# Layer one's first unit in another order on three engines, and a later wait for the low parts of the weight sums

## The chip, the cores and the metric

The kernel runs on one core of one Trainium2 chip. The metric is the device time of one execution in microseconds. Engines are named as in the profile: PE is TensorE (PEld its weight loads), DVE is VectorE, ACT is ScalarE, POOL is GpSimd, SP issues the DMAs.

## The reference

A hash-bucketed attention (2 batches, 8 heads, 768 tokens, head size 64), then two gated MLPs.

```python
def _attn_ref(q, k, v, proj):
    ...
    mask = q_bucket[:, :, :, None] == k_bucket[:, :, None, :]
    scores = np.where(mask, scale * q @ k.T, -1e9)
    attn = exp(scores - max); attn = attn / (sum(attn) + 1e-09)
    return attn @ v
def _moe_ref(x, w1, w2, w3, w_out):        # 1536 x 512, width 1024
    return ((x @ w1) * (x @ w2) @ w3) @ w_out
def _moe2_ref(x, w_gate, w_val, w_out):    # 1536 x 512, width 1536
    return (sigmoid(x @ w_gate) * (x @ w_val)) @ w_out
```

All is float32. The kernel splits each float32 operand into a high part (rounded to the matmul's format, fp32r) and a low part (the rest), and makes each product from three matmuls: high by high, low by high, high by low.

## The kernel before, in words

The work has four stages: attention over eight pairs of heads (0 to about 281 us), layer one (`x @ w1` and `x @ w2`, gated, to about 404 us), layer two (w3 times w_out), and layer three with the last product (to 746.9 us).

Layers one and three use a Strassen-like scheme with seven products for each 2 x 2 block of blocks. A unit is one block column of one weight matrix: `unit(pair, j)` with j = 0 for the first matrix and j = 1 for the second. Seven products follow each other, each for two sides (halves of the tokens): B11, T3, T2, T1, B22, B21, T4, named after the operand from x. B names are blocks of x, T names are sums of blocks. The product of one side is six matmuls of 128x384. Each product needs the operand's high and low part and the weight's high and low part. The weights A11, A12, A22 are raw blocks; S1 to S4 are sums of blocks. B11, B21 and T4 use raw blocks, T3, T2, T1 and B22 use sums.

Around the first unit the order is written out by hand, with counting semaphores:

- GpSimd, for each unit, runs `pair_sums` (four sums, L549 to L557), `pair_raw_low` (L562, signals `g_raw_split`) and `pair_sums_low` (L567, signals `g_ready`). For unit 1 this follows its last work for attention, the low parts of B22 (L634). `pair_sums(1, 1)` waits for the weights' load and for the last attention-side product of weights (`wp_done`).
- ScalarE runs `pair_raw_high` and `pair_sums_high` for the weights' high parts, `x_operand_high` for the operands' high parts, and `kept1`, `kept2`, `kept4`, which copy a bank of partial results to memory after the products B11, T2 and T1. TensorE waits for the copy of one side before it goes on in the same bank (T2, T1 and B22 wait for `u1_kept`, `u2_kept`, `u4_kept`). Its order for the first unit stands from L868 to L887.
- VectorE makes the operands' low parts (`x_operand_low`, L1070, two inputs in SBUF, signals `x_ready`), the last attention results (`attention_out`, L1054), the sums for T4 (`x_sum4_begin`, `x_sum4`) and, within `unit`, adds a bank to a kept part (L1184). The T3 low parts stand at the end of the last pair (L1128, L1129), ahead of the last `transposed_lo` (L1048), which makes `pt_lo`. The order behind stands from L1164 to L1178. The T4 low parts follow the first two adds of unit 0 (L1232).
- TensorE ends attention with the last value products, whose last twelve matmuls (`values`, L1351) stand between B11 and T3 of the first unit; they need all `pt_lo`. At its start a unit waits for `g_ready`, that is for all low parts of its weights.
- SP loads the next weights (`load_pair`, L424) when GpSimd has finished the raw low parts of the unit before.

Of the kernel before, what the change touches and what calls it, by code (L numbers as in the profile page):

```python
# [65 lines left out]
B11, T3, T2, T1, B22, B21, T4 = range(7)  # L66
# [4 lines left out]
X_LOW_ORDER = ((T3, 0), (T3, 1), (T2, 0), (T2, 1), (T1, 0), (T1, 1), (B21, 0), (B21, 1), (T4, 0), (T4, 1))  # L71
# [9 lines left out]
def build(nc, qk_d, v_d, proj_d, shift_d, w1_d, w2_d, w3_d, wo1_d, wg_d, wv_d, wo2_d, out_d):  # L81
    ctx = ExitStack()
    with ctx:
# [117 lines left out]
        u_x, u_y = kept_parts(1, (86, 89, 92)), kept_parts(3, (134, 137, 161))  # L201
# [57 lines left out]
        x_hi_done, x_ready = sem("x_hi_done"), sem("x_ready")  # L259
# [218 lines left out]
        def _(pool):  # L478
# [63 lines left out]
            def pair_sums(unit, j):  # L542

                sums = g_sum[j]
                pool.wait_ge(g_loaded, 48 * (unit + 1))
                at_least(pool, w2_mm, 2 * (unit - 1))
                if isinstance(unit, int) and unit == 1:
                    pool.wait_ge(wp_done, PAIRS)
                pool.tensor_tensor(sums[:, S1 - S1, :], g_raw21[:, 0, :], g_raw[:, A22, :],  # L549
                                   ALU.add).then_inc(g_sums_done, 1)  # L550
                pool.tensor_tensor(sums[:, S3 - S1, :], g_raw[:, A11, :], g_raw21[:, 0, :],
                                   ALU.subtract).then_inc(g_sums_done, 1)
                pool.wait_ge(g_sums_done, 4 * unit + 1)
                pool.tensor_tensor(sums[:, S2 - S1, :], sums[:, S1 - S1, :], g_raw[:, A11, :],
                                   ALU.subtract).then_inc(g_sums_done, 1)
                pool.wait_ge(g_sums_done, 4 * unit + 3)
                pool.tensor_tensor(sums[:, S4 - S1, :], g_raw[:, A12, :], sums[:, S2 - S1, :],  # L557
                                   ALU.subtract).then_inc(g_sums_done, 1)
# [126 lines left out]
        def _(act):  # L685
# [3 lines left out]
            def pair_raw_high(unit, j):  # L689

                act.wait_ge(g_loaded, 48 * (unit + 1))
                at_least(act, w2_mm, 2 * (unit - 1))
                if isinstance(unit, int) and unit == 1:
                    act.wait_ge(wp_done, PAIRS)
                copy(g_hi[j][:, A11:S1, :], g_raw[:, :, :]).then_inc(g_raw_hi_done, 1)
# [5 lines left out]
            def x_operand_high(q, side):  # L701

                if q == T1:
                    act.wait_ge(s_done, STEPS * PAIRS)
                if q in (T2, T1):
                    act.wait_ge(x_sums_done, {T2: 3, T1: 5}[q] + side)
                    act.wait_ge(s_done, STEPS * (PAIRS - 1) + QT)
                if q == B21:
                    act.wait_ge(wp_done, PAIRS)
                    act.wait_ge(x_done, 2 * PAIRS - 1 + 2 * side)  # L710
                if q == T4:
                    act.wait_ge(x_sum4_begun, 1)
                    act.wait_ge(x_sum4_done, side + 1)
                copy(x_high(q, side), x_raw(q, side)).then_inc(x_hi_done, 1)
# [114 lines left out]
            def kept2(pair, j, side, u):  # L829
                kept(pair, j, side, y2_mm, u2_kept, u[1], g21_done, v21_done)  # L830

            def kept4(pair, j, side, u):
                kept(pair, j, side, y3_mm, u4_kept, u[2], g22_done, v22_done)
# [33 lines left out]

            x_take_t2()  # L868
            kept1(0, 0, 0, u_x)
            pair_raw_high(1, 1)  # L870
            kept1(0, 0, 1, u_x)
            x_operand_high(T1, 1)
            attention_halves(3, PAIRS - 1, keep=False)
            kept2(0, 0, 0, u_x)
            x_operand_high(B21, 0)
            kept2(0, 0, 1, u_x)
            x_operand_high(B21, 1)
            kept4(0, 0, 0, u_x)
            kept4(0, 0, 1, u_x)
            x_operand_high(T4, 0)  # L880
            x_operand_high(T4, 1)
            for side in range(2):
# [113 lines left out]
        def _(dve):  # L996
# [103 lines left out]
            def pair(p, first=False, last=False):  # L1100
                for k in range(STEPS):
                    nxt = None if last and k == STEPS - 1 else (p, k + 1) if k + 1 < STEPS else (p + 1, 0)
                    if nxt:
                        row_max(*nxt)
                    if last:
                        sum_eps(p, k)
                    if nxt:
                        exp_scale(*nxt)
                    if last:
                        inverse(p, k)  # L1110
                    if nxt:
                        exp_bias(*nxt)
                    if last and k not in NORM_ON_ACT:
                        normalise(p, k)
                    if k == 0 and not first:
                        sums_eps_of(p - 1, 1)
                    if k > 0:
                        transposed_lo(p, k - 1)
                    elif not first:
                        inverse_of(p - 1)  # L1120
                        transposed_lo(p - 1, STEPS - 1)
                        turn(p - 1)
                    if k == QT and not last:
                        sums_eps_of(p, 0)
                    if k == (4 if first else 2) and not last:
                        code(p + 1)
                    if last and k == STEPS - 1:
                        x_operand_low(T3, 0)  # L1128
                        x_operand_low(T3, 1)  # L1129

            dve.memset(inverses[:, :], 0.0).then_inc(pad_set, 1)
            dve.wait_ge(pad_set, 1)
# [29 lines left out]
                pair(p)  # L1162
            pair(PAIRS - 1, last=True)
            transposed_lo(PAIRS - 1, STEPS - 1)  # L1164
            x_sum4_begin()
            x_operand_low(T2, 0)
            x_operand_low(T2, 1)
            dve.wait_ge(x_kept, 4 * PAIRS - 1)
            attention_out(slice(0, 2 * D), 0, x_f[:, PAIRS - 1, 0:HALF])
            x_sum4(0)  # L1170
            x_operand_low(T1, 0)
            x_operand_low(T1, 1)
            attention_out(slice(0, D), 1, x_f[0:D, PAIRS - 1, HALF:SEQ])
            dve.wait_ge(x_tmp_done, 4 * PAIRS)
            attention_out(slice(D, 2 * D), 1, pv_bank[D:2 * D, 0:HALF])
# [130 lines left out]
        def _(pe):  # L1306
# [129 lines left out]
            def unit(pair, j, high, low, operand=None, behind_first=()):  # L1436


                n = 4 * pair + 2 * j
                pe.wait_ge(g_ready, 2 * pair + j + 1)  # L1440
                if operand:
                    pe.wait_ge(g_raw_split, 2 * pair + j + 1)

                def ready(q, side):
                    if operand:
                        operand(q, side)

                for side in range(2):
                    ready(B11, side)
                    if j == 1:  # L1450
                        pe.wait_ge(g12_done, 2 * pair + side + 1)
                    elif not isinstance(pair, int) or pair > 0:
                        pe.wait_ge(v12_done, 2 * pair + side - 1)
                    product(j, A11, high(B11, side), low(B11, side), y_bank[side], True, y1_mm)
                for go, *args in behind_first:
                    go(*args)
                for side in range(2):
                    ready(T3, side)
                    at_least(pe, c21_done, n + side - 1)
                    product(j, S3, high(T3, side), low(T3, side), w_bank[side], True, w1_mm)  # L1460
                for side in range(2):
                    ready(T2, side)
                    pe.wait_ge(u1_kept, n + side + 1)
                    product(j, S2, high(T2, side), low(T2, side), y_bank[side], False, y2_mm)
                for side in range(2):
                    ready(T1, side)
                    pe.wait_ge(u2_kept, n + side + 1)
                    product(j, S1, high(T1, side), low(T1, side), y_bank[side], False, y3_mm)
                for side in range(2):
                    ready(B22, side)  # L1470
                    pe.wait_ge(u4_kept, n + side + 1)
                    product(j, S4, high(B22, side), low(B22, side), y_bank[side], False, y4_mm)
                for side in range(2):
                    ready(B21, side)
                    at_least(pe, c11_done, n + side - 1)
                    product(j, A12, high(B21, side), low(B21, side), x_bank[side], True, x_mm)
                for side in range(2):
                    ready(T4, side)
                    pe.wait_ge(c22_done, n + side + 1)
                    product(j, A22, high(T4, side), low(T4, side), w_bank[side], False, w2_mm)  # L1480
# [136 lines left out]
```

## Time and profile before

| | us |
|---|---|
| median of 3 runs | 747.89 (747.79 to 748.35) |
| the profiled execution | 748.67 |
| its span | 746.9 |

| engine | busy, us | share of the span |
|---|---|---|
| TensorE | 726.1 | 97% |
| VectorE | 435.8 | 58% |
| ScalarE | 432.3 | 58% |
| GpSimd | 363.8 | 49% |

The span runs from the first to the last instruction of the profiled execution. Granted TensorE clock is 0.995 of full speed over the span. A row of a timeline gives the start and the duration of an instruction, or of several of one kind merged (x2), and in brackets how long its engine was idle before and what ended that. Matmuls overlap, so the distance from one start to the next is what one costs.

### The profile page before, as it was taken

The page shows a single profiled execution, that of the slowest core. Times are in us where ns is not written, and L with a number is a line of the kernel's source. Part 1 is how long each engine was busy: PE and PEld are TensorE (multiplying, and loading weights), DVE is VectorE, ACT ScalarE, POOL GpSimd, SP SyncE. Part 2 cuts the span into 40 slices and gives each one's busy share as a digit, 9 for nine tenths or more (in the row PEclk, how much of TensorE's full clock was granted, in tenths as well). Part 3 has the DMA queues.
Part 4 walks back from the last instruction along what each step waited for, and adds up shares of the span by engine and source line. Part 5 has one row for each costly group of instructions (what it writes and reads, how often), then busy time and mean ns, then how long its engine had stood idle before and what let it go on. Part 6 is the DMA issues. An engine that isn't in the chain of part 4 may idle for free.

```text
span 746.9 us, 12529 instructions
## 1 busy us (share of the span) xinstructions
PE 726.1 (97%) x4120; PEld 675.8 (90%) x4120; DVE 435.8 (58%) x837; ACT 432.3 (58%) x819; POOL 363.8 (49%) x308
## 2 busy tenths in 40 slices
PE   6899999999999889999999999999999999999998
PEld 4789898988989778999999999999999999988886
DVE  5879889898888989415336345541441434855100
ACT  5978888888888887463454434635336355705100
POOL 3897658375578794564358100255446534320000
PEclk9899999999999999999999999999999999999999
DMA  4665465554566100001110000001000100501001
GB/s 131 189 187 156 114 166 150 132 159 126 142 157 135 32 29 28 29 29 57 28 29 29 1 1 1 29 29 52 33 28 29 57 28 6 163 1 70 29 29 42
DMA packets 28003, 53.43 MB, mean 72 GB/s; under 512 B 4976, under 2 KB 13504, under 8 KB 27968
## 3 DMA queue, kind: packets, MB, share of 16 engines
q1 hardware_dynamic: 27664, 52.94, 25.8%
q8 instruction: 17, 0.28, 0.1%
q14 instruction: 18, 0.15, 0.1%
q10 hardware_dynamic: 304, 0.07, 0.0%
HBM read 32.18 MB, written 3.19 MB: 47 GB/s over the span
## 4 chain that ended last, share of the span: by engine, by line
PE 81%; DVE 9%; ACT 4%; issue 3%; DMA 1%; POOL 1%; DVEq 0%; ACTq 0%; SPq 0%
PE pair_bank L1423 14%; PE pair_bank L1425 14%; PE pair_bank L1424 14%; PE bank L1425 6%; PE bank L1424 6%; PE bank L1423 6%; PE bank L1336 6%; PE pair_bank L1321 5%; PE bank L1351 5%; DVE rowmax L1000 2%; DVE pt_lo L1048 2%; PE bank L1385 2%; PE bank L1384 2%; PE bank L1386 2%; ACT prob L727 1%
## 5 line engine op out<-in xcount | busy, mean ns | idle before, releaser
L1184 DVE TENSOR_TENSOR u<-bank,u 128x384 f32<-128x384 f32 x80 | 44.3, 555 | 136.0 <-ACT u L687 126.3
L687 ACT ACTIVATE u<-pair_bank 128x384 f32<-128x384 f32 x120 | 58.7, 491 | 107.0 <-PE pair_bank L1425 107.0
L1048 DVE TENSOR_TENSOR pt_lo<-bank,pt_hi 128x384 fp32r<-128x384 f32 x192 | 97.6, 550 | 24.2 <-ACT pt_hi L687 23.6
L727 ACT ACTIVATE prob<-pair_bank,ebias,escale 128x768 f32<-128x768 f32 x96 | 95.7, 997 | 9.3 <-DVE ebias L1011 9.3
L687 ACT ACTIVATE pt_hi<-bank 128x384 fp32r<-128x384 f32 x192 | 83.8, 488 | 29.5 <-PE bank L1336 29.0
L1321 PE MATMUL pair_bank<-mk,sq 128*128 128x384 f32 x384 | 93.0, 365 | 2.7 <-ACT prob L727 2.5
L1000 DVE TENSOR_REDUCE rowmax<-pair_bank 128x1 f32<-128x768 f32 x96 | 90.7, 945 | 2.9 <-PE pair_bank L1321 2.8
L1336 PE MATMUL bank<-ident,prob 128*128 128x128 f32 x576 | 83.2, 279 | 6.1 <-DVE pt_lo L1048 5.0
L1336 PEld LDWEIGHTS bank<-ident,prob 128*128 128x128 f32 x576 | 67.6, 142 | 22.1 <-DVE pt_lo L1048 5.8
L1423 PE MATMUL pair_bank<-y_hi,g_hi 128*128 128x384 f32 x240 | 80.2, 334 | 0.0
L549 POOL TENSOR_TENSOR g_sum<-g_raw,g_raw 128x256 f32<-128x256 f32 x20 | 18.0, 898 | 110.5 <-PE bank L1425 110.5
L1321 PEld LDWEIGHTS pair_bank<-mk,sq 128*128 128x128 f32 x384 | 63.8, 194 | 8.3 <-issue 4.4
L562 POOL TENSOR_TENSOR g_raw_lo<-g_raw,g_hi 128x768 fp32r<-128x768 f32 x20 | 38.2, 1910 | 65.1 <-ACT g_hi L687 65.1
L1351 PE MATMUL bank<-pt_hi,v_st 128*128 128x384 f32 x192 | 64.9, 338 | 0.9 <-issue 0.7
L1351 PE MATMUL bank<-pt_lo,v_st 128*128 128x384 f32 x192 | 64.6, 337 | 0.0
L1423 PE MATMUL pair_bank<-x_hi,g_hi 128*128 128x384 f32 x160 | 53.9, 337 | 1.8 <-ACT u L687 1.3
L567 POOL TENSOR_TENSOR g_sum_lo<-g_sum,g_hi 128x1024 fp32r<-128x1024 f32 x20 | 47.9, 2393 | 10.0 <-ACT g_hi L687 10.0
L1425 PE MATMUL pair_bank<-y_hi,g_sum_lo 128*128 128x384 f32 x144 | 48.1, 334 | 0.0
L1424 PE MATMUL pair_bank<-b_lo,g_hi 128*128 128x384 f32 x144 | 48.1, 334 | 0.0
L1424 PE MATMUL pair_bank<-wo_lo,gv_hi 128*128 128x512 f32 x120 | 46.7, 389 | 0.0
L1425 PE MATMUL pair_bank<-wo_hi,gv_lo 128*128 128x512 f32 x120 | 46.7, 389 | 0.0
L1423 PE MATMUL pair_bank<-wo_hi,gv_hi 128*128 128x512 f32 x120 | 46.7, 389 | 0.0
(170 smaller groups left out, 1889.6 us busy)
## 6 DMA issues: line engine op xcount, KB each, us to landing
sq<-hl SPq DMA_DIRECT2D x42, 192.0 KB
qk_raw<-in_qk SPq DMA_DIRECT2D x7, 768.0 KB, 5.7
mk<-hl SPq DMA_DIRECT2D x14, 384.0 KB
w_raw<-in_w SPq DMA_DIRECT2D x16, 256.0 KB, 2.7
v_raw<-in_v SPq DMA_DIRECT2D x16, 192.0 KB, 2.7
wo_raw<-in_wo SPq DMA_DIRECT2D x12, 256.0 KB, 3.7
out<-out_sb SPq DMA_DIRECT2D x12, 256.0 KB, 2.0
mk<-hl SPq DMA_DIRECT2D x14, 192.0 KB
```

The source lines that it names most:

```text
L567: pool.tensor_tensor(g_sum_lo[j][:, :, :], g_sum[j][:, :, :], g_hi[j][:, S1:7, :].bitcast(F32), ALU.subtract).then_inc(g_ready, 1)
L687: return act.activation(dst, src, ACT.Copy)
L727: act.activation(prob[k % 3][:, :].rearrange("p (c n) -> p c n", c=KC), pair_bank[k % 2][:, :, 0:HALF], ACT.Exp, bias=ebias[:, k:k + 1], s ...
L1000: dve.tensor_reduce(rowmax[:, k:k + 1], pair_bank[k % 2][:, :, 0:HALF], AX.XY, ALU.max).then_inc(max_done, 1)
L1048: dve.tensor_tensor(pt_lo[(k // UQ) % 2][cut], t_bank[j][:, 0:384].rearrange("p (t n) -> p t n", t=3), pt_hi[(k // UQ) % 2][cut].bitcast(F ...
L1184: dve.tensor_tensor(acc, src, acc, ALU.add).then_inc(done, 1)
L1321: mm = pe.matmul(pair_bank[k % 2][:, kc, 0:HALF], sq[hd][:, part, q0:q0 + 128], mk[hd][:, part, HALF * kc:HALF * kc + HALF], start=(part = ...
L1336: mm = pe.transpose(t_bank[j][:, 128 * t:128 * t + 128], prob[k % 3][:, 128 * (3 * j + t):128 * (3 * j + t) + 128], ident[:, :])
L1351: mm = pe.matmul(pv_bank[:, 0:HALF], v_st[hd][:, kt, :], moving[slot][:, kt, :], start=(kt == 0 and moving is pt_hi), stop=(kt == QT - 1 a ...
L1423: pe.matmul(dst, hi, m_hi, start=start, stop=False, skip_group_check=partial)
L1424: pe.matmul(dst, hi, m_lo, start=False, stop=False, skip_group_check=partial)
L1425: return pe.matmul(dst, lo, m_hi, start=False, stop=stop, skip_group_check=partial)
```

## The change

Four places change. VectorE: the low part T3 of side 1 moves behind the last `transposed_lo`, and the two T1 low parts move ahead of `attention_out`. GpSimd: the sums of unit 1 wait until `x_ready` counts the low part T1 of side 1. ScalarE: `pair_raw_high(1, 1)` moves from behind the first `kept1` to behind both `kept2`, the high part T1 of side 1 moves ahead of the second `kept1`, and the high parts of B21 move behind both `kept2` and behind both `kept4`. TensorE: every unit waits at its start for `g_raw_split` alone and for `g_ready` before its second product, T3.

```diff
 def pair_sums(unit, j):            # GpSimd
     if isinstance(unit, int) and unit == 1:
         pool.wait_ge(wp_done, PAIRS)
+        pool.wait_ge(x_ready, X_LOW_ORDER.index((T1, 1)) + 1)
 ...                                # ScalarE
 x_take_t2()
 kept1(0, 0, 0, u_x)
-pair_raw_high(1, 1)
+x_operand_high(T1, 1)
 kept1(0, 0, 1, u_x)
-x_operand_high(T1, 1)
 attention_halves(3, PAIRS - 1, keep=False)
 kept2(0, 0, 0, u_x)
+kept2(0, 0, 1, u_x)
+pair_raw_high(1, 1)
 x_operand_high(B21, 0)
-kept2(0, 0, 1, u_x)
-x_operand_high(B21, 1)
 kept4(0, 0, 0, u_x)
 kept4(0, 0, 1, u_x)
+x_operand_high(B21, 1)
 x_operand_high(T4, 0)
 x_operand_high(T4, 1)
 ...                                # VectorE
         if last and k == STEPS - 1:
             x_operand_low(T3, 0)
-            x_operand_low(T3, 1)
 ...
 transposed_lo(PAIRS - 1, STEPS - 1)
+x_operand_low(T3, 1)
 x_sum4_begin()
 x_operand_low(T2, 0)
 x_operand_low(T2, 1)
+x_operand_low(T1, 0)
+x_operand_low(T1, 1)
 dve.wait_ge(x_kept, 4 * PAIRS - 1)
 attention_out(slice(0, 2 * D), 0, x_f[:, PAIRS - 1, 0:HALF])
 x_sum4(0)
-x_operand_low(T1, 0)
-x_operand_low(T1, 1)
 attention_out(slice(0, D), 1, x_f[0:D, PAIRS - 1, HALF:SEQ])
 ...                                # TensorE, unit()
-pe.wait_ge(g_ready, 2 * pair + j + 1)
-if operand:
-    pe.wait_ge(g_raw_split, 2 * pair + j + 1)
+pe.wait_ge(g_raw_split, 2 * pair + j + 1)
 ...                                # B11, both sides
 for go, *args in behind_first:
     go(*args)
+pe.wait_ge(g_ready, 2 * pair + j + 1)
 for side in range(2):
     ready(T3, side)
```

## Rows read from the trace of the kernel before

**Rows 1.** The page, part 1: busy us, share of the span, instructions.

```profile
PE 726.1 (97%) x4120; PEld 675.8 (90%) x4120; DVE 435.8 (58%) x837; ACT 432.3 (58%) x819; POOL 363.8 (49%) x308
```

**Rows 2.** Waits of TensorE, 280 to 320 and 300 to 746 us: total, times, longest.

```profile
PE pair_bank L1423 <- ACT u L687: 0.9, 1, 0.9
...
PE pair_bank L1423 <- DVE x_sum_lo L1070: 0.5, 1, 0.5
...
PE pair_bank L1423 <- DVE h_lo L1229: 0.6, 1, 0.6
```

**Rows 3.** Timeline of TensorE, first unit: start, duration, instruction.

```profile
281.63 0.35 PE L1423 MATMUL pair_bank<-x_hi,g_hi 128*128 128x384 f32 x1
...
284.03 0.45 PE L1351 MATMUL bank<-pt_hi,v_st 128*128 128x384 f32 x1
...
288.30 0.33 PE L1423 MATMUL pair_bank<-x_hi,g_hi 128*128 128x384 f32 x1
...
290.21 0.34 PE L1425 MATMUL pair_bank<-x_hi,g_sum_lo 128*128 128x384 f32 x1
291.07 0.44 PE L1423 MATMUL pair_bank<-x_hi,g_hi 128*128 128x384 f32 x1 [0.52 <-DVE x_sum_lo L1070]
...
294.40 0.41 PE L1423 MATMUL pair_bank<-x_hi,g_hi 128*128 128x384 f32 x1 [0.95 <-ACT u L687]
...
300.73 0.44 PE L1423 MATMUL pair_bank<-x_hi,g_hi 128*128 128x384 f32 x1
```

**Rows 4.** Timeline of VectorE, 279 to 299 us.

```profile
279.94 3.11 DVE L1070 TENSOR_TENSOR x_lo<-x_f,x_hi 128x768 fp32r<-128x768 f32 x2
...
283.90 1.25 DVE L1078 TENSOR_TENSOR x_sum<-x_f,x_sum 128x768 f32<-128x768 f32 x1
285.35 3.74 DVE L1070 TENSOR_TENSOR x_sum_lo<-x_sum,x_hi 128x768 fp32r<-128x768 f32 x2 [0.20 <-DVE x_sum L1078]
289.01 0.54 DVE L1054 TENSOR_TENSOR x_f<-x_f,x_tmp 128x384 f32<-128x384 f32 x1
...
290.06 1.82 DVE L1070 TENSOR_TENSOR x_sum_lo<-x_sum,x_hi 128x768 fp32r<-128x768 f32 x2
...
293.44 1.82 DVE L1070 TENSOR_TENSOR x_lo<-x_f,x_hi 128x768 fp32r<-128x768 f32 x2
...
296.24 1.81 DVE L1070 TENSOR_TENSOR x_sum_lo<-x_sum,x_hi 128x768 fp32r<-128x768 f32 x2
```

**Rows 5.** The chain that ended last, 280 to 300 us.

```profile
286.49 2.60 DVE x_sum_lo L1070
```

**Rows 6.** Timeline of GpSimd, 278 to 301 us.

```profile
278.99 1.83 POOL L634 TENSOR_TENSOR x_lo<-x_f,x_hi 128x768 fp32r<-128x768 f32 x1
...
284.40 1.34 POOL L557 TENSOR_TENSOR g_sum<-g_raw,g_sum 128x256 f32<-128x256 f32 x1
285.71 2.56 POOL L562 TENSOR_TENSOR g_raw_lo<-g_raw,g_hi 128x768 fp32r<-128x768 f32 x1
298.27 2.40 POOL L567 TENSOR_TENSOR g_sum_lo<-g_sum,g_hi 128x1024 fp32r<-128x1024 f32 x1 [10.00 <-ACT g_hi L687]
```

**Rows 7.** GpSimd's last sum and raw low parts, all units: ns min/median/max.

```profile
L557 POOL TENSOR_TENSOR g_sum<-g_raw,g_sum x20: 734/739/1340, 233.0 to 620.0; 128x256 f32<-128x256 f32 x20
...
L562 POOL TENSOR_TENSOR g_raw_lo<-g_raw,g_hi x20: 1842/1846/2558, 262.3 to 621.0; 128x768 fp32r<-128x768 f32 x20
```

**Rows 8.** Timeline of ScalarE, 280 to 299 us.

```profile
280.80 0.88 ACT L687 ACTIVATE pt_hi<-bank 128x384 fp32r<-128x384 f32 x2
...
284.11 0.84 ACT L687 ACTIVATE g_hi<-g_raw 128x768 fp32r<-128x768 f32 x1
...
289.54 0.49 ACT L687 ACTIVATE u<-pair_bank 128x384 f32<-128x384 f32 x1 [2.63 <-PE pair_bank L1425]
...
293.78 0.86 ACT L687 ACTIVATE u<-pair_bank 128x384 f32<-128x384 f32 x2
...
297.14 1.05 ACT L687 ACTIVATE g_hi<-g_sum 128x1024 fp32r<-128x1024 f32 x1
```

## The prediction

> **What bounds the kernel now.** I read the page first. TensorE is busy for 97% of the span [rows 1], so a change elsewhere counts only where it makes or removes a pause of TensorE. The list of waits comes next, once for the stretch of layer one's first unit and once for everything behind it. The reader is to see that the first unit has two pauses of TensorE, one that ends on a low part made by VectorE and one that ends on a copy made by ScalarE, and that from 300 us to the end there are only two more, 0.4 us in layer one's last unit and 0.6 at the start of layer two, of which the longer is shown [rows 2]. TensorE's own timeline puts places to them. A product of one side is six matmuls: the first of twelve starts at 288.30 and the last at 290.21, so one costs 0.1736 us, a product 1.04 and a pair of sides 2.08. The first unit starts at 281.63 and the second at 300.73. Between lie 14 products and twelve matmuls of attention values, 16 x 1.04 = 16.66, against 19.10 elapsed: 2.44 us are pauses. They are 0.30 before the values (284.03), 0.69 before T1 (291.07), 1.11 before B22 (294.40), and about 0.1 behind each, where the first matmul takes 0.41 to 0.45 and not 0.33 [rows 3]. Nothing behind runs on a fixed time: each later unit's work on the other engines starts from TensorE's semaphores. What moves the second unit's start moves the end of the kernel.
>
> VectorE, ScalarE and GpSimd are then read as timelines of the same 20 us. In VectorE's, two low parts of one kind take 1.82 us where GpSimd is idle, which is 0.95 each with the next one let in 0.08 before the end (0.87 from start to start). The T3 pair took 3.11 and the T2 pair 3.74 [rows 4], and the second of T2 alone 2.60 [rows 5]. GpSimd shows the other half: its last sum takes 1.34 where the median of that line is 0.74, and its raw low parts 2.56 where the median is 1.85 [rows 6, 7]. Fitted together the ends say that only one of the two runs. The raw low parts end at 288.27 and VectorE's low part at 289.09, 0.82 later. VectorE's x_sum ends at 285.15 and GpSimd's sum at 285.74, 0.59 later, and the next low part 0.83 after that. GpSimd's raw low parts end 1.70 after this. When both are waiting, they take turns [rows 4 to 6].
>
> The Trainium skill ("SBUF — State Buffer", Who interferes with whom) says the same sharply: a tensor_tensor of VectorE with both inputs in SBUF and a GpSimd instruction that reads SBUF exclude each other for a whole instruction, and the one that starts first wins; it rejects a split of bandwidth. A duration of 2.60 by itself would fit a split too. The sum below is for turns, a split is a rival.
>
> **The change, part by part.**
> (a) VectorE turns the low part T3,1 behind the last pt_lo pair. T3,0 still starts at 279.94 behind GpSimd's x_lo, which ends at 280.82, and ends at 281.63. The last transposed halves leave ScalarE at 281.3 and 281.7 (unchanged), so the pt_lo pair ends at 282.6 and no longer behind 283.9 [rows 4, 8]. The values need it at 283.74. The 0.30 pause and its 0.11 go.
> (b) GpSimd's four sums for unit 1 wait until T1,1 is ready. VectorE is then alone: T3,1 from 282.50, x_sum4_begin 283.37 to 284.32, T2,0 from 284.52 (its wait on x_sum costs 0.20 as now), T2,1 285.39, T1,0 286.26, T1,1 287.13 to 288.08. TensorE asks for T2 at 287.90 and 288.94, T1 at 289.98 and 291.02. All are in time: the 0.69 pause and its 0.11 go. For T1,1 ScalarE's high part moves before the second kept1, 284.1 to 284.95.
> (c) ScalarE. TensorE's T2,0 at 287.90 gives the copy kept2 at 289.14 (288.30 to 289.54 now, 1.24) and the second at 290.18. A 384 copy lets the next in 0.39 after its start, a 768 copy 0.73 [rows 8]. pair_raw_high(1, 1) starts 290.57, the high part B21,0 291.30, kept4 292.04 to 292.52. TensorE is at B22 at 292.06 and starts 0.14 behind the copy, as it does now (294.26, 294.40): 292.66. The 1.11 pause becomes 0.60. Here TensorE is 1.74 us ahead of before. Behind follow kept4 (292.42), B21,1 (292.81 to 293.65), T4,0 and T4,1 (to 295.12), two gates from 295.02 and 295.41, and pair_sums_high(1, 1) 295.80 to 296.85 [rows 8]. ScalarE has no gap in it.
> (d) What GpSimd now does later. Its sums enter at 288.16, beside the attention_out and x_sum4 instructions of VectorE, which ran with GpSimd idle before. In turns: VectorE's 384 instruction (0.54; blocked, I put it at 0.41 behind the release, as the 768 one loses 0.13) ends 288.54; sum 289.13; 289.54; sum 290.13; 290.54; sum 291.13; VectorE, one from PSUM and one from SBUF, to 291.73; last sum 292.32. Its raw high part has been ready since 291.41. B21,0 (high part ready at 292.14) then ends 293.14, the raw low parts 294.84, and B21,1 at 295.66. If GpSimd wins the turn before B21,0, the same three end by 295.8. TensorE asks for B21 at 294.82 and 295.86: just in time.
> (e) T4. The two adds between B21 and T4 take 0.98 (295.26 to 296.24 now), so T4,0 starts 296.64 and ends 297.59. GpSimd's sums' low parts, 2.40 alone [rows 6], enter at 296.93, 0.08 behind ScalarE. Before, they started at 298.27, after both T4 low parts were done at 298.05. Now they take the turn between them: 297.59 + 2.25 = 299.84, and T4,1 ends 300.66. TensorE asks for T4,0 at 296.90 and gets it at 297.65; it asks for T4,1 at 298.79 and gets it at 300.72. It ends the unit at 300.72 + 1.04 + 0.1 = 301.86. Before: 300.73. That is +1.13; the 0.11 to 0.13 lost at the start of unit 1 now (first matmul 0.44, its weights had just come at 300.67) [rows 3, 6] goes, because this unit now waits for the raw low parts alone there. Sum: +1.0 us.
> (f) The sums' low parts asked for at the second product. In unit 1 they are ready at 299.84 and asked for at 303.9. In all later units no pause ends on them [rows 2], and the wait added stands among waits before each product that cost nothing: 0. Bounds: 0 to 0.1 us a unit, the price of a restart, if it did not hide; I take 0, since the waits before the other products show no gap now.
> (g) The load of the next g_raw waits for the raw low parts: issued 294.9 and not 288.44; landing in under 3 us, wanted only when T4 is done at 302: 0.
>
> I take +1.1 us (the sum, and a little for the order of turns, which can only add). The profiled execution took 748.67 us, of which 746.9 are its span and 1.8 lie around it; it is 0.8 above the median 747.89. The difference goes onto the median: **749.0 us**.
>
> **Rivals.**
> 1. T4,1 gets through before the sums' low parts. VectorE would have to reach it by 296.93 and not 297.51, 0.6 sooner. Then no pause is left but the 0.60: unit 1 starts at 298.98, -1.75, and with its 0.13 -1.9 us: 746.0. For it: if attention_out and the sums did not block each other, the sums would end at 291.1, the raw low parts at 293.3, B21,1 at 295.0 and T4,1 would start at 296.86, 0.07 in time. Against: both inputs of these are in SBUF, as in every blocked pair of [rows 4 to 6]. It decides the sign, with its place at 296.9.
> 2. The low parts of the sums start before T4,0 (0.3 us apart): 299.33, T4,0 300.15, T4,1 301.02, unit 1 at 302.3: +1.5, 749.4.
> 3. A split and not turns: at half speed each, T4,0 ends 298.3 and T4,1 300.0, unit 1 at 301.2: +0.3 to +0.4, 748.3. Small shifts that let only part of this through fall here too. Against: the ends fit turns within 0.02.
> 4. The hold on GpSimd does nothing, because something else stretches T2: against it speaks that T1's pair takes 1.82 as soon as GpSimd is idle [rows 4, 6]. T1 would keep its 0.8, and with (e) that is about +1.9. I give it no chance of its own.
>
> **Numbers.** Likeliest case 0.55, own range 748.6 to 749.5; rival 1 0.20, rival 2 0.10, rival 3 0.15. The bound of 0.2%, about what can be told from no change, is 1.5 us: below 746.4 or above 749.4. Rival 1 is faster: 0.20. Slower takes half or more of rival 2 and the upper tail of the likeliest, where one more turn goes to GpSimd: 0.20. The rest is 0.60. Leaving rival 1 out would leave over 0.2 outside, so the range reaches to it: 745.9 to 749.7.
>
> **What would show it.** Right: the list of waits of TensorE has no low part of x_sum before T1 and a pause of about 0.6 on ScalarE's copy before B22; T2's low parts take 0.95; GpSimd's four sums start at about 288.2 and are stretched; and in front of T4,1 stands a pause of near 2 us that ends on VectorE, whose T4 pair takes over 3.5 us while GpSimd's g_sum_lo overlaps it. Wrong: the T4 pair at 1.8 us (rival 1, and the kernel is faster), or T4,1 stretched by about 1.5 us with g_sum_lo stretched beside it (rival 3).

## The result, and the profile after

| | before | changed |
|---|---|---|
| median of 11 runs | 747.79 (747.11 to 748.35) | 749.05 (748.03 to 750.80) |
| profiled execution, its span | 748.67, 746.9 | 748.03, 746.2 |
| first unit's start to second's, us | 281.63 to 300.73: 19.10 | 279.96 to 300.18: 20.22 |
| second unit's start to the end | 446.2 | 446.0 |

The changed kernel takes 1.0021 times as long, 95% interval 1.0013 to 1.0028, that is +1.0 to +2.1 us; the medians are 1.26 apart. (Two runs far outside all others, 1839.63 us of e1 below and 2531.17 of the kernel before beside e1 to e4, are in no ratio.) The two spans point the other way, and this is the first thing to read right: the changed kernel's profiled execution is the fastest of its eleven, and it came out of attention 1.67 us earlier (279.96 against 281.63). The granted clock in attention differs between the two: 0.66 in two 5 us windows from 15 to 25 us before, 1.00 in the changed kernel. That this makes the 1.67 is not shown: e11 below, the changed kernel with 0.96 and 0.70 there, starts its first unit at 280.40, and e9 with 1.00 at 280.62. e6, the kernel before with TensorE's waits alone edited, has 0.56 and 0.76 from 15 to 25 us and starts it at 280.60. The distance in time to the first unit differs from one execution to the next, whatever the edit. From the first unit's first matmul to the end it is 465.27 us before and 466.24 changed: +0.97. The distance between the two units' starts is the measure that follows the change, and I use it throughout. Behind the second start 0.1 to 0.15 is won back, which the old kernel lost there on a slow first matmul [rows 3].

TensorE's waits in the changed kernel, 270 to 746 us (total, times, longest):

```profile
PE bank L1424 <- DVE x_sum_lo L1071: 2.3, 2, 1.7
PE pair_bank L1424 <- ACT u L688: 0.8, 2, 0.4
...
PE pair_bank L1424 <- DVE h_lo L1230: 0.6, 1, 0.6
```

T1's wait of [rows 2] is gone and ScalarE's 0.9 is 0.4, but VectorE's low parts now cost 2.3 in two waits. TensorE's timeline puts them in front of both sides of T4:

```profile
279.96 0.35 PE L1424 MATMUL pair_bank<-x_hi,g_hi 128*128 128x384 f32 x1
...
290.98 0.41 PE L1424 MATMUL pair_bank<-x_hi,g_hi 128*128 128x384 f32 x1 [0.43 <-ACT u L688]
...
295.99 0.44 PE L1424 MATMUL bank<-x_hi,g_hi 128*128 128x384 f32 x1 [0.58 <-DVE x_sum_lo L1071]
...
299.03 0.45 PE L1424 MATMUL bank<-x_hi,g_hi 128*128 128x384 f32 x1 [1.71 <-DVE x_sum_lo L1071]
...
300.18 0.33 PE L1424 MATMUL pair_bank<-x_hi,g_hi 128*128 128x384 f32 x1
```

From start to start, less the 0.17 of a matmul, the pauses are 0.60 (B22), 0.75 (T4,0) and 1.88 (T4,1), each with about 0.1 behind it. Their cause is in the timelines of VectorE and GpSimd:

```profile
282.83 3.57 DVE L1071 TENSOR_TENSOR x_sum_lo<-x_sum,x_hi 128x768 fp32r<-128x768 f32 x4 [0.20 <-DVE x_sum L1079]
...
286.91 0.98 DVE L1087 TENSOR_TENSOR x_sum<-x_f,x_sum 128x384 f32<-128x384 f32 x1
287.81 1.09 DVE L1055 TENSOR_TENSOR x_f<-x_f,x_tmp 64x384 f32<-64x384 f32 x1
...
291.98 2.03 DVE L1071 TENSOR_TENSOR x_lo<-x_f,x_hi 128x768 fp32r<-128x768 f32 x1 [0.49 <-ACT x_hi L688]
...
294.98 3.99 DVE L1071 TENSOR_TENSOR x_sum_lo<-x_sum,x_hi 128x768 fp32r<-128x768 f32 x2
```

```profile
286.57 0.89 POOL L550 TENSOR_TENSOR g_sum<-g_raw,g_raw 128x256 f32<-128x256 f32 x1 [7.42 <-DVE x_sum_lo L1071]
...
289.57 1.10 POOL L558 TENSOR_TENSOR g_sum<-g_raw,g_sum 128x256 f32<-128x256 f32 x1
290.63 2.57 POOL L563 TENSOR_TENSOR g_raw_lo<-g_raw,g_hi 128x768 fp32r<-128x768 f32 x1
295.20 2.96 POOL L568 TENSOR_TENSOR g_sum_lo<-g_sum,g_hi 128x1024 fp32r<-128x1024 f32 x1 [2.00 <-ACT g_hi L688]
```

The four low parts of T2 and T1 take 3.57 together, where the T2 pair alone took 3.74 [rows 4]. The price comes at T4: the T4 pair takes 3.99 and not 1.81, since GpSimd's low parts of the sums came up at 295.20, while T4,0 ran, and were next when it ended.

### The profile page after: what moved, and what is told of

It reads as the page before. It is cut to its first block, busy times and chain, and to the rows that moved or that the text cites. A ratio compares the mean times of both kernels' runs of the same rounds, so it can differ in the third digit from the quotient of the medians.

```text
span 746.2 us, 12539 instructions
## 1 busy us (share of the span) xinstructions
PE 722.7 (97%) x4120; PEld 672.4 (90%) x4120; DVE 436.6 (59%) x837; ACT 431.7 (58%) x819; POOL 364.9 (49%) x308
## 4 chain that ended last, share of the span: by engine, by line
PE 83%; DVE 9%; ACT 4%; issue 3%; POOL 1%; DMA 1%; DVEq 0%; SPq 0%; ACTq 0%
PE pair_bank L1424 14%; PE pair_bank L1426 14%; PE pair_bank L1425 14%; PE bank L1337 6%; PE pair_bank L1322 6%; PE bank L1352 6%; PE bank L1424 6%; PE bank L1426 6%; PE bank L1425 6%; DVE pt_lo L1049 2%; DVE rowmax L1001 2%; PE bank L1385 2%; PE bank L1386 2%; PE bank L1387 2%; ACT pt_hi L688 1%
## 5 line engine op out<-in xcount | busy, mean ns | idle before, releaser
L1322 PE MATMUL pair_bank<-mk,sq 128*128 128x384 f32 x384 | 91.0, 359 | 4.2 <-ACT prob L728 4.0
L1322 PEld LDWEIGHTS pair_bank<-mk,sq 128*128 128x128 f32 x384 | 62.1, 189 | 9.6 <-ACT prob L728 5.2
```

The lines of the kernel that those rows point to most:

```text
L1322: mm = pe.matmul(pair_bank[k % 2][:, kc, 0:HALF], sq[hd][:, part, q0:q0 + 128], mk[hd][:, part, HALF * kc:HALF * kc + HALF], start=(part = ...
```

## The experiments

All ratios are to the kernel before, run beside each on the same chip, with 95% intervals; its median was 747.96 beside e1 to e4, 747.62 beside e5, e6 and e8, and 747.87 beside e12. "Distance" is from the first unit's first matmul to the second's. The edits are to the changed kernel, where nothing else is said. The line numbers of their rows are shifted by the edits.

**e1: the sums' low parts behind T4,1.**

```diff
 def pair_sums_low(unit, j):
     pool.wait_ge(g_sums_hi_done, unit + 1)
+    if isinstance(unit, int) and unit == 1:
+        pool.wait_ge(x_ready, X_LOW_ORDER.index((T4, 1)) + 1)
```

> The changed kernel with one wait more: GpSimd makes the low parts of unit 1's weight sums only when VectorE has finished the low part T4 of side 1. The measure is the distance from the first matmul of the first unit to that of the second: 19.10 us before (and 0.13 lost behind it), 20.22 changed. Theory of turns: T4's two low parts take 1.8 us and not 3.99, the wait of 1.7 us before T4,1 goes, the sums' low parts start near 297 and are done before the second product wants them. Distance 18.2, so 2.0 us less than the changed kernel and 0.9 to 1.0 less than before: ratio 0.9987. Rival, the stretched T4 pair comes from something else (ScalarE's high parts, or a split of bandwidth that only partly costs): distance 19.5 to 20.2, ratio 1.000 to 1.002.

Measured: distance 18.22, ratio 0.9984 (0.9975 to 0.9993), median 746.85. Before T4,1 no pause is left; before T4,0 it is 0.73. In VectorE's and GpSimd's timelines the T4 pair is back at 1.82 and g_sum_lo at 2.41:

```profile
295.86 1.82 DVE L1073 TENSOR_TENSOR x_sum_lo<-x_sum,x_hi 128x768 fp32r<-128x768 f32 x2
```

```profile
297.82 2.41 POOL L570 TENSOR_TENSOR g_sum_lo<-g_sum,g_hi 128x1024 fp32r<-128x1024 f32 x1 [3.75 <-DVE x_sum_lo L1073]
```

One wait added on GpSimd gives back 2.0 us, as expected from turns. The meeting at T4 is shown as the cause of the loss.

**e7: the same wait one low part earlier.** As e1 with `(T4, 0)` for `(T4, 1)`, a single run.

> As e1, but GpSimd's sums' low parts wait for the low part T4,0 and not T4,1, so they come up just as T4,0 ends, when VectorE has let T4,1 in 0.08 us earlier. Turns, the one that is in first goes first and whole: the T4 pair takes 1.82 as in e1, GpSimd's g_sum_lo is stretched from 2.40 to about 3.2, distance 18.2. A split of bandwidth: T4,1 is stretched too, the pair takes 2.5 or more, and g_sum_lo about 3.2 as well. GpSimd first: the pair takes 4.1, distance 20.2.

Measured: distance 18.25. GpSimd now comes up at the end of T4,0, when T4,1 has just been let in:

```profile
295.56 1.82 DVE L1073 TENSOR_TENSOR x_sum_lo<-x_sum,x_hi 128x768 fp32r<-128x768 f32 x2
```

```profile
296.65 3.00 POOL L570 TENSOR_TENSOR g_sum_lo<-g_sum,g_hi 128x1024 fp32r<-128x1024 f32 x1 [2.88 <-DVE x_sum_lo L1073]
```

VectorE loses nothing. GpSimd's instruction takes 3.00 where it took 2.41 in e1 (I had put it at 3.2): it alone pays for the overlap. A split of bandwidth would have stretched both. It fell.

**e2: no hold on the sums.**

```diff
     if isinstance(unit, int) and unit == 1:
         pool.wait_ge(wp_done, PAIRS)
-        pool.wait_ge(x_ready, X_LOW_ORDER.index((T1, 1)) + 1)
```

> The changed kernel without the wait of GpSimd on the low part T1: its four sums for unit 1 start at once beside VectorE's low parts, the raw low parts stay late because ScalarE's high part is late. Theory of turns: T2 and T1 come about 1 us later, still in time for TensorE, but GpSimd's raw low parts end some 0.5 us earlier, and the T4 pair comes close to getting through before the sums' low parts: either as in the changed kernel (distance 20.0 less 0.5, 19.5) or, if T4,1 starts first, 17.7 to 18.0. Rival, that the hold is what makes T1 timely: the wait of 0.5 before T1 comes back and the distance is 20.5 or more.

Measured: distance 19.82, ratio 1.0014 (1.0005 to 1.0022). No wait before T1; T4,0 pauses 0.36, T4,1 still 1.90. I expected 19.5: the T4,0 pause shrank by 0.4, not 0.5 or more, and T4,1 still loses its race: GpSimd's low parts of the sums come up while T4,0 runs.

**e3: no hold, and the sums' low parts behind T4,1** (e1 and e2 together).

> The changed kernel without the wait on T1 and with the sums' low parts behind T4,1. Turns: no wait before T1, 0.6 before B22, 0.2 before T4, distance 17.5 to 17.7, that is 1.5 us less than before, ratio 0.9980. If the hold on T1 is needed, a wait of 0.5 or more before T1 and a distance of 18.2 or more.

Measured: distance 17.80 (expected 17.5 to 17.7: T4,0 pauses 0.34 and not 0.2), ratio 0.9981 (0.9972 to 0.9990), median 746.43. The hold on T1 is not needed: T1 is in time without it. It even costs: the distance is 0.42 shorter without it than in e1, and 0.40 shorter in e2 than in the changed kernel, nearly all of it in the pause before T4,0.

**e4: TensorE's wait for g_ready at the unit's start again.** The change's edit in `unit` of TensorE undone.

> The changed kernel with TensorE's waits as before: a unit asks for the sums' low parts at its start. They are done at 298.2 in the changed kernel's trace and its second unit starts at 300.18, so this costs nothing there: distance 20.2, ratio to before 1.0015 to 1.002. Rival, that the wait in the middle of all 20 units is part of the loss: ratio 1.001 or less.

Measured: distance 20.22, ratio 1.0018 (1.0009 to 1.0028). The second unit's first matmul is not slow here either:

```profile
300.13 0.33 PE L1424 MATMUL pair_bank<-x_hi,g_hi 128*128 128x384 f32 x1
```

In the changed kernel the later wait neither costs nor gives anything that could be seen.

**e6: the kernel before with that edit alone.**

> The kernel before with TensorE's waits of the change alone: g_ready before the second product of each unit. Forecast: only the slow first matmul at the start of unit 1 goes, 0.03 in the distance of the first unit and 0.11 behind it: ratio 0.9998 to 1.000, not to be told from no change. Rival, a wait in the middle of 20 units costs 0.05 to 0.1 us each: 1 to 2 us slower, ratio 1.0013 to 1.0027.

Measured: distance 19.05 and no slow first matmul behind it, ratio 1.0000 (0.9991 to 1.0009). A wait in the middle of every unit costs nothing that can be seen: the interval is 0.7 us either way for 20 units, and from the second unit's start to the end it is 446.0 with such waits (changed, e6) and 446.0 without (e4).

**e8: the kernel before with ScalarE's order alone.** The diff's ScalarE part, nothing else.

> The kernel before with ScalarE's new order alone; VectorE's order, no hold on GpSimd and TensorE's waits as before. Turns: GpSimd's raw low parts come near 291.5 of before's time and not at 285.7, so the T2 pair is not stretched and the wait of 0.69 before T1 goes; the 1.11 before B22 becomes 0.6. The T4 pair and the sums' low parts then come within 0.1 us of each other: if T4,1 is first, distance 18.0 to 18.2 and ratio 0.9987; if not, 19.8 to 20.1 and ratio 1.001. Rival, only VectorE's new order makes T1 timely: a wait before T1 of 0.5 or more stays.

Measured: distance 18.82 (expected 18.0 to 18.2), ratio 0.9999 (0.9990 to 1.0008) and not 0.9987. In VectorE's timeline the T2 pair takes 2.08 and the T4 pair 1.82:

```profile
284.21 2.08 DVE L1070 TENSOR_TENSOR x_sum_lo<-x_sum,x_hi 128x768 fp32r<-128x768 f32 x2 [0.20 <-DVE x_sum L1078]
...
295.23 1.82 DVE L1070 TENSOR_TENSOR x_sum_lo<-x_sum,x_hi 128x768 fp32r<-128x768 f32 x2
```

T1's wait is gone without VectorE's new order and without the hold, so it was the raw low parts' place, set by `pair_raw_high`, that had stretched T2. T4,1 won its race, but I had left out who loses it: GpSimd's low parts of the sums. They end at 299.31, and the unit of this kernel asks for them at its start. GpSimd's row, and TensorE's first matmul of the second unit:

```profile
296.15 3.16 POOL L567 TENSOR_TENSOR g_sum_lo<-g_sum,g_hi 128x1024 fp32r<-128x1024 f32 x1 [3.57 <-ACT g_hi L687]
```

```profile
299.36 0.44 PE L1423 MATMUL pair_bank<-x_hi,g_hi 128*128 128x384 f32 x1 [0.74 <-POOL g_sum_lo L567]
```

By this, the later wait for g_ready would be worth the 0.9 of the pause here; that is an estimate, since no run has ScalarE's order and the later wait alone.

**e12: the kernel before with VectorE's order alone.**

> The kernel before with VectorE's new order alone: T3,1 behind the last pt_lo, T1 ahead of attention_out. GpSimd's sums and its raw low parts (high part early, as before) stay beside VectorE's low parts. Turns: the 0.30 before the values goes; each of T3,1, x_sum, T2 and T1 waits for one GpSimd instruction, and the high part T1,1 stands behind the second kept1, so T2,1 comes 0.2 late and T1,1 about 1.4, and B22 waits some 0.4 less than 1.11; distance 18.9 to 19.2, ratio 0.9997 to 1.0001. Rival, VectorE's order is by itself what makes T1 timely: no wait before T1, distance 18.3 or less, ratio 0.999.

Measured: distance 19.09, ratio 0.9998 (0.9989 to 1.0007), pauses 0.22 before T2,1, 1.40 before T1,1, 0.53 before B22, as expected. But the size came out right with half of its reason wrong. ScalarE's timeline has the rest:

```profile
291.55 0.84 ACT L687 ACTIVATE x_hi<-x_f 128x768 fp32r<-128x768 f32 x1 [1.78 <-DVE x_f L1054]
292.30 0.47 ACT L687 ACTIVATE u<-pair_bank 128x384 f32<-128x384 f32 x1
```

The low part T1,1 was ready at 290.98, 1.9 us before TensorE took it up at 292.92. What TensorE waited for is the second kept2 at 292.30, in line behind the high part B21,0, which itself waited 1.78 us for attention_out on VectorE, now behind the T1 low parts. So VectorE's new order gains nothing without ScalarE's (19.09 against 19.10): with kept2 ahead of B21,0, as in the change, that wait has nothing to hold up.

**e5: a better order.** Built on e3.

```diff
 def pair_raw_low(unit, j):
     pool.wait_ge(g_raw_hi_done, unit + 1)
+    if isinstance(unit, int) and unit == 1:
+        pool.wait_ge(x_ready, X_LOW_ORDER.index((B21, 1)) + 1)
 ...
 attention_halves(3, PAIRS - 1, keep=False)
+pair_raw_high(1, 1)
 kept2(0, 0, 0, u_x)
 kept2(0, 0, 1, u_x)
-pair_raw_high(1, 1)
 x_operand_high(B21, 0)
 kept4(0, 0, 0, u_x)
-kept4(0, 0, 1, u_x)
 x_operand_high(B21, 1)
+kept4(0, 0, 1, u_x)
```

> Built on e3: GpSimd's sums start at once and its sums' low parts wait for T4,1; in addition the raw low parts wait for B21,1, ScalarE's pair_raw_high stands in its gap before kept2, and the high part B21,1 stands between the two kept4. Turns: the 0.6 before B22 goes, since kept4 has only one high part ahead of it, B21's low parts no longer meet the raw low parts, and the wait before T4 falls to 0.1 to 0.2. Distance 16.9 to 17.1 (e3 17.80), so 2.1 to 2.3 us less than before: ratio 0.9972. If the wait before B22 or T4 hangs on something else than these two, it stays near 17.8.

Measured: distance 17.09, with one pause of 0.30 (T4,0), and the pause before B22 gone; the profiled execution's span is 743.3, the shortest of all. The median is 746.59, ratio 0.9988 (0.9979 to 0.9997). By the ratios it beats both kernels, but 0.9972 was expected and lies outside the interval: the distance says 2.0 us less than before, the medians 1.0. Its trace is 0.7 us ahead of e3's and its ratio is not; they ran on different chips, and its eleven runs spread over 2.4 us where e3's spread over 1.1. Where the 0.7 goes in the slower runs I did not see: open.

**e9 to e11: the changed kernel run three times more.**

> The changed kernel as it is, looked at again. Its eleven runs reach from 748.0 to 750.8 us, and so do those of e2 and e4, the other two with a pause of TensorE of 1.9 us before T4,1 (747.8 to 750.6, 747.9 to 751.1), while e1, e3, e6 and e8 stay within 1.4 us of their fastest. Theory: in some executions the granted clock falls behind that pause and comes back some microseconds later, which costs 1.5 to 2.5 us; in a slow execution's trace the clock in a window behind 299 us is below 1.00 and the stretch from the second unit's start to the end is longer than the 446.0 us of the first profile. Rival: the spread comes from the attention stage, so the first unit starts later than 281.7 and the stretch behind it is 446.0.

> A second look at the changed kernel, with the same expectations as e9: if its time is above 749.4, either the clock in a window behind the pause before T4,1 is below 1.00 and the stretch from the second unit's start to the end exceeds 446.0 us by the excess, or the first unit starts later than 281.7. In a time below 748.6 neither is seen. The distance between the units' starts is 20.2 in both.

> A third look at the changed kernel, as e9 and e10: a time above 749.4 comes with a low clock behind the pause (theory) or with a late start of the first unit (rival), and the distance between the two units' starts is 20.2 us in each.

Measured: 748.66, 748.46 and 750.05. The pauses are the same in all three (0.60, 0.70 to 0.77, 1.88 to 1.90), the first unit starts at 280.62, 280.45 and 280.40, and the distance is 20.20, 20.21 and 21.16. The third shows in TensorE's timeline that the matmuls behind the pause come 0.32 apart and not 0.17:

```profile
299.48 0.69 PE L1424 MATMUL bank<-x_hi,g_hi 128*128 128x384 f32 x1 [1.72 <-DVE x_sum_lo L1071]
299.96 0.53 PE L1425 MATMUL bank<-x_sum_lo,g_hi 128*128 128x384 f32 x1
...
302.52 0.52 PE L1424 MATMUL pair_bank<-x_hi,g_hi 128*128 128x384 f32 x1
...
303.24 0.34 PE L1424 MATMUL pair_bank<-x_hi,g_hi 128*128 128x384 f32 x1
```

and the stage windows, first of e11, then of e10, show the granted clock (the third column from the right), the share of full speed:

```profile
295.00:299.00 4.00, 2.15 (x11) 1.51 (x9) 4.00 (x4) 1.37 (x3) 2.98 (x1) 1.00 0.36 125
299.00:301.00 2.00, 1.52 (x5) 1.52 (x6) 1.82 (x4) 1.07 (x3) 0.00 (x0) 0.62 0.03 8
301.00:303.00 2.00, 2.00 (x8) 2.00 (x7) 0.56 (x1) 0.98 (x3) 1.15 (x2) 0.52 0.00 0
303.00:305.00 2.00, 2.00 (x13) 2.00 (x12) 0.00 (x0) 1.40 (x4) 1.71 (x3) 1.00 0.00 0
```

```profile
299.00:301.00 2.00, 1.49 (x8) 1.49 (x9) 2.00 (x5) 1.05 (x3) 0.10 (x1) 1.00 0.00 0
301.00:303.00 2.00, 2.00 (x13) 2.00 (x13) 0.41 (x1) 1.87 (x5) 2.00 (x3) 1.00 0.00 0
```

The twelfth matmul of the second unit starts 23.73 us behind the first unit's start in e11 and 22.11 in e10: the clock at its lower level, 1.2 GHz, cost 1.6 us. That is the difference of the two times. The rival, a late start of the first unit, fell for this execution: 280.40 is the earliest of the three. The theory held for the execution seen. What the expectation got wrong is its measure: the clock fell at the end of the pause, so part of the loss is in the distance itself, which I had put at 20.2 in each.

## Why the prediction was right, point by point

The median was forecast at 749.0 and is 749.05. By its own steps, with the changed kernel's own times moved by the 1.67 us that it came out of attention earlier:

| step of the prediction | forecast | measured |
|---|---|---|
| (a) pause before the values | 0 | 0 |
| (b) pause before T1 | 0 | 0 |
| (b) GpSimd's sums start | 288.16 | 286.57, that is 288.24 |
| (c) pause before B22 | 0.60 | 0.60 |
| (d) B21,0 and B21,1 ready | 293.14, 295.66 | 291.49 and 294.01, that is 293.16 and 295.68 |
| (e) pauses before T4,0 and T4,1 | 0.75, 1.93 | 0.75, 1.88 |
| (e) distance | +1.13 | +1.12 |
| (e) sum | +1.0 | +0.97 |
| (f) later wait for g_ready, in the changed kernel | 0 | 0 (e4) |
| (g) later load of the next weights | 0 | 0: GpSimd's first sum for the unit behind waits for TensorE's bank, not for a load |

The reading that carried it was that of [rows 4 to 6]: one VectorE instruction of 2.60 us beside one GpSimd instruction of 2.56 is two instructions in turn and not two slow ones. With that, a list of who comes up when is enough, and it gave each number within 0.1 us. The page of the Trainium skill ("SBUF — State Buffer", Who interferes with whom) that rules out a split is borne out by e7 (VectorE's pair 1.82 as alone, GpSimd 3.00 and not 2.41).

Two reasons given in the prediction are not those that the runs show, though the times came. Step (b) has T2 and T1 in time because GpSimd is held back. In e2, e3 and e8 nothing holds the sums back, and there is no wait before T1: the later place of the raw low parts is enough. In this rival 4 had its first half right; T1 did not keep its 0.8, because ScalarE's order took it away. Step (e) lets the slow first matmul of unit 1 go because the unit no longer asks for the sums' low parts at its start. In the changed kernel these are done at 298.16 and the unit starts at 300.18, and e4, which asks for them at the start, has no slow first matmul.

What was not in it is the clock. I took +1.1, and the traces say +0.97 for the mechanism; the medians are 1.26 apart. The rest, 0.3, lies within the interval of the ratio, and I put it down to executions like e11's, in which TensorE's clock fell behind the new pause of 1.9 us. Five of the changed kernel's eleven runs lie above 749.4, four of e2's twelve and four of e4's eleven; no run of the kernel before or of e1, e3, e5, e6, e8 or e12 that is in a ratio does. e2 and e4 are the other two with this pause. The mean granted clock of each run fits: it is 0.993 or 0.991 in five of these thirteen, and 0.995 or more in every other run for which it is on record. The other eight have 0.995, as some quick runs have from a low stretch in attention and as e11 has, so in them this figure decides nothing. The clock's fall is shown in one execution; that it makes all of that tail is argued from this pattern. So the closeness of 749.0 is partly luck: a smaller mechanism with an unforeseen one on top, and a kernel before whose median came out 0.1 lower (747.79) than the 747.89 that the forecast started from. Four single runs lie above the range's end of 749.7, which was given for the median.

Rival 1 did not come: GpSimd's low parts of the sums came up at 295.20, while T4,0 ran. What it would have given was not measured in the changed kernel. e1 and e3 (746.85, 746.43) have no pause before T4,1 either, but keep 0.73 and 0.34 before T4,0, which the rival's 746.0 does not have. e8 shows who pays when T4,1 wins by itself: the sums' low parts, and with them a unit that asks for them at its start. The changed kernel asks later, so the rival's price could leave that out; my expectation for e8 could not, and did.

Rival 3, the split, had 0.15 and fell to e7. Rival 2 did not come: T4,0 was first by 0.2 us (294.98 against 295.20).

What the change bought and lost, then: the new orders took away 1.72 us of pauses and restarts (0.41 at the values, 0.80 at T1, 0.51 at B22) and, by holding GpSimd's sums back from about 279 to 286.5 (in the changed kernel's times) and the raw high part to behind kept2, brought GpSimd's last two instructions into the one place where VectorE had no slack. 2.85 us were given back there (0.75 and 1.88, 0.11 behind each), which leaves +1.13 in the distance.

## What to carry to other kernels

Where VectorE reads two operands from SBUF, write its instructions and GpSimd's on one line of time, one at a time, and ask of each that TensorE waits for: which GpSimd instruction comes up while its forerunner runs? The dear case is a short pair with a long GpSimd instruction between them; a wait that holds the long one until the pair is done cost nothing here and gave 2.0 us.

To hold an engine back frees the place where it was and crowds the place where it goes; follow it to its last instruction before judging the edit. Here the hold on the sums was not needed and cost 0.4 us.

Where the forecast is a us in 750, compare stretches within a trace, from the first matmul that the change touches: spans of single executions here pointed the wrong way.

## What the hardware showed that I had not expected

TensorE's granted clock fell to its lower level behind a pause of 1.9 us that followed one of 0.75 us 3 us earlier, in one of four traces of the same kernel with the same pauses, and stayed there until 302.9 (0.62 and 0.52 of full speed in two windows of 2 us). In the other three it was 1.00 throughout the stretch, and so it was in the traces of e2 and e4, which have the same pause of 1.9 us.

The turns of VectorE and GpSimd are exact enough to add up. A blocked 128x768 low part of VectorE ends 0.82 us behind GpSimd's instruction, and GpSimd's blocked sum 0.59 behind VectorE's [rows 4 to 6]; in e7 the first to come up ran whole at its lone duration.
